# Row loads ahead of result stores, an earlier copy of the first Strassen product, and a second block weighted tile by tile

## What is computed

```python
ret = scores * Dmat                       # scores = q k^T / 8, a decay per head, lower triangle
x = (ret @ v), tokens x 512               # 4 batches, 8 heads, 576 positions, 64 wide
logits = x @ w_gate + log1p(exp(x @ w_noise)) * noise
top2 = argpartition(-logits, 2)[:, :2]    # top2_w = softmax over the two
out[mask] += top2_w * (relu(x[mask] @ w1[e]) @ w2[e])     # 8 experts, hidden width 1024
h = out @ w_in                            # 512 x 2048
y = (h * cos(h)) @ w_out                  # 2048 x 512
```

## Time and profile before

| what | value |
|---|---|
| median of 3 runs | 984.74 us (984.18 to 987.29) |
| the profiled execution | 986.97 us, its span 985.2 us |
| PE / PEld busy | 959.6 us (97%) / 860.7 us (87%) |
| DVE / ACT / POOL busy | 562.3 us (57%) / 477.7 us (48%) / 94.7 us (10%) |
| chain that ended last | PE 75%, SP's queue 6%, DMA 5%, ACT 5%, DVE 4% |
| moved | 231.92 MB, mean 235 GB/s |

### The profile page before, as it was taken

How to read it: one execution, slowest core, us unless ns; L and a number is a source line. 1 busy time by engine, 2 the same in 40 slices (tenths; PEclk the granted TensorE clock), 3 DMA queues, 4 the chain that set the end, 5 groups by cost and what they waited for, 6 DMA issues and landing times.

```text
span 985.2 us, 17024 instructions
## 1 busy us (share of the span) xinstructions
PE 959.6 (97%) x6144; PEld 860.7 (87%) x6144; DVE 562.3 (57%) x1118; ACT 477.7 (48%) x889; POOL 94.7 (10%) x93
## 2 busy tenths in 40 slices
PE   8999999999999999999999999999999999999998
PEld 8888889898988989899998988988988888788887
DVE  4788644544545554433332145567777767776665
ACT  1445334343433443332333146556767766666555
POOL 2276500000000000000000032101100000000000
PEclk9999999999999999999999999999999999999999
DMA  9998455468688786764526248867764766556561
GB/s 364 345 321 303 173 203 202 160 236 310 262 270 329 265 322 229 256 248 150 192 67 231 86 137 304 289 252 289 265 240 167 291 256 235 184 216 249 228 235 54
DMA packets 79521, 231.92 MB, mean 235 GB/s; under 512 B 6880, under 2 KB 32736, under 8 KB 71264
## 3 DMA queue, kind: packets, MB, share of 16 engines
q1 hardware_dynamic: 73696, 212.20, 60.2%
q0 software_dynamic: 5760, 18.88, 5.2%
HBM read 168.14 MB, written 62.91 MB: 235 GB/s over the span
## 4 chain that ended last, share of the span: by engine, by line
PE 75%; SPq 6%; DMA 5%; ACT 5%; DVE 4%; issue 3%; POOL 1%; DVEq 0%; ACTq 0%; POOLq 0%
PE ps L1855 16%; PE ps L1666 13%; PE ps L1684 13%; PE ps L1841 12%; SPq L539 4%; PE ps L1771 3%; PE ps L1783 2%; PE ps L1819 2%; PE ps L1572 2%; PE ps L1610 2%; DMA gath<-x_slots 2%; PE ps L1587 2%; DMA y_slots<-y_sb 2%; PE ps L1638 2%; PE ps L1702 2%
## 5 line engine op out<-in xcount | busy, mean ns | idle before, releaser
L1666 PE MATMUL ps<-xs,w_hi 128*128 (+1 forms) x784 | 185.3, 316 | 0.0
L1855 PE MATMUL ps<-w_sb,g_hi 128*128 128x512 f32 x576 | 180.8, 395 | 0.1
L1272 DVE TENSOR_TENSOR w_lo<-raw,w_hi 128x1024 fp32r<-128x1024 f32 x48 | 58.8, 1226 | 159.2 <-ACT w_hi L794 159.2
L1666 PEld LDWEIGHTS ps<-xs,w_hi 128*128 128x128 f32 x784 | 135.3, 191 | 0.7
L1666 PE MATMUL ps<-xs,w_lo 128*128 (+1 forms) x392 | 122.5, 312 | 0.0
L1841 PE MATMUL ps<-x_odd,w_sb 128*128 128x320 f32 x672 | 118.7, 312 | 3.9 <-DVE angle L1442 1.8
L1841 PEld LDWEIGHTS ps<-x_odd,w_sb 128*128 128x128 f32 x672 | 107.4, 189 | 15.8 <-ACT p_sb L935 3.4
L794 ACT ACTIVATE w_hi<-raw 128x1024 fp32r<-128x1024 f32 x48 | 50.9, 1060 | 136.6 <-PE ps L1684 107.5
L1855 PE MATMUL ps<-w_sb,g_lo 128*128 128x512 f32 x288 | 112.7, 391 | 0.0
L1855 PEld LDWEIGHTS ps<-w_sb,g_hi 128*128 128x128 f32 x576 | 101.3, 188 | 9.8 <-issue 0.3
L716 POOL DMA_INDIRECT y<-y_slots,pos_i x36 | 34.9, 970 | 636.3 <-SPq L636 446.1
(11 more groups left out here) (193 smaller groups left out, 1615.8 us busy)
## 6 DMA issues: line engine op xcount, KB each, us to landing
w_sb<-w_pairs SPq DMA_DIRECT2D x24, 1792.0 KB
w_sb<-w_pairs SPq DMA_DIRECT2D x40, 1024.0 KB, 9.7
raw<-weights SPq DMA_DIRECT2D x64, 512.0 KB
w_pairs<-stage SPq DMA_DIRECT2D x24, 1024.0 KB, 7.1
y_slots<-zeros_sb SPq DMA_DIRECT2D x42, 256.0 KB, 4.1
gath<-x_slots SPq DMA_DIRECT2D x40, 256.0 KB, 7.1
y_slots<-y_sb SPq DMA_DIRECT2D x40, 256.0 KB, 2.1
qk<-qk SPq DMA_DIRECT2D x18, 512.0 KB
```

The source lines that it names most:

```text
L1272: tt(w_lo[:, at], raw[:, f % 2, :], w_hi[:, at].bitcast(F32), ALU.subtract).then_inc(split_done, 1)
L1666: last_one = nc.tensor.matmul(ps[5 + half][:, 0:HALF], w[:, at:at + P], xs[:, bass.ds(g % 2, 1), a, k, half * HALF:(half + 1) * HALF].rear ...
L1855: last_one = nc.tensor.matmul(ps[j][:, :], a[:, slot % 2, part, j * C:(j + 1) * C], w2_sb[slot % 3][:, hl, part * DM:(part + 1) * DM], sta ...
```

## The change

On SP, `unit_loads(g)` now starts with the two value loads, then issues the loads of the next unit's rows 0 and 1, then the five stores of unit g - 1, and then the rest. The stores of the last unit of the loop follow behind it. In units 2 to 6 the value loads and two row loads thus stand between the zero blocks of the unit before and its stores.

On ACT, `copy_p1` stands ahead of `cosine(slot - 1, 3)`, no more behind it, and `x2_high(1, 6)` moves from slot 7 to slot 8, behind `copy_p1(8)`; `x2_low(1, 6)` moves behind the first drain of slot 8. The first product of slot 8 gets the bank ps[7], and the banks of the later products change places, so that products 1 and 2 of slot 8 wait for the last two cosine products of block 0.

The first three tiles of block 1 are weighted one by one around `turn(1, 1)` and `cosine(1, 1)` on ACT and inside slot 2 on DVE, and PE transposes them in the middle of slot 2, behind the first `plain` of that slot and its `second` steps, no more ahead of it.

```diff
--- before.py
+++ after.py
@@ -329,7 +329,9 @@
 
         def p_bank(i):
 
-            return ps[7] if i == 2 else ps[5 + i % 2]
+            if i in (2, 2 * FP):
+                return ps[7]
+            return ps[5 + (i + (i > 2 * FP)) % 2]
 
         def x_of(b):
 
@@ -573,14 +575,17 @@
                 else:
                     sp.dma_start(w2_pairs[i], stage2[i % 2][:, :, :].bitcast(F32)).then_inc(pair_out[i % 2], 16)
 
-            for j in range(TPU):
-                store_rows(0, j)
-
             def unit_loads(g):
                 e_next = nc.sync.value_load(meta[0:1, bass.ds(g + 1, 1)], min_val=0, max_val=E - 1)
                 v_next = nc.sync.value_load(meta[0:1, bass.ds(g + META_V + 1, 1)], min_val=0, max_val=NV - 1)
+                for j in range(2):
+                    sp.wait_ge(tx_done, TPU * g + j + 1)
+                    sp.sem_inc(passed_sp, 1)
+                    load_rows(j, v_next)
+                for j in range(TPU):
+                    store_rows(g - 1, j)
                 for f in range(FE):
-                    if f < TPU:
+                    if 2 <= f < TPU:
                         sp.wait_ge(tx_done, TPU * g + f + 1)
                         sp.sem_inc(passed_sp, 1)
                         load_rows(f, v_next)
@@ -600,14 +605,12 @@
                 unit_loads(g)
                 for j in range(E):
                     zero_block(E * TPU + j + (g - 1) * E)
-                for j in range(TPU):
-                    store_rows(g, j)
             sp.wait_ge(zero_out, 16 * (TPU * (NU - E) + TPU - FRONT[1]))
             sp.sem_inc(passed_sp, 1)
             with sp.Fori(E - 2, last) as g:
                 unit_loads(g)
-                for j in range(TPU):
-                    store_rows(g, j)
+            for j in range(TPU):
+                store_rows(last - 1, j)
 
             def load_w1(slot):
                 if slot >= 2:
@@ -971,9 +974,6 @@
             def ahead(b, p):
                 first = FIRST_TILE[b + 1]
                 if b == 0:
-                    if p == 1:
-                        for j in range(3):
-                            prepare(first + j)
                     if p == 2:
                         for j in range(3):
                             copy_raw(first + j)
@@ -990,8 +990,6 @@
                     if p == 6:
                         for at in range(3, 6):
                             x2_high(1, at)
-                    if p == 7:
-                        x2_high(1, 6)
                 else:
                     if 1 <= p <= 5:
                         copy_raw(first + p - 1)
@@ -1015,17 +1013,24 @@
                 g_high(slot, 0)
                 ahead(0, slot)
                 turn(slot, 1)
+                if slot == 1:
+                    prepare(FIRST_TILE[1])
                 cosine(slot, 1)
+                if slot == 1:
+                    prepare(FIRST_TILE[1] + 1)
+                    prepare(FIRST_TILE[1] + 2)
             for slot in range(FP, SLOTS + 1):
                 b, p = slot // FP, slot % FP
                 if slot == FP:
                     g_high(slot - 1, 1)
+                    if slot < SLOTS:
+                        copy_p1(slot)
+                    x2_high(1, 6)
                 else:
                     g_high(slot - 1, 2)
+                    if slot < SLOTS:
+                        copy_p1(slot)
                     cosine(slot - 1, 3)
-                if slot < SLOTS:
-                    copy_p1(slot)
-                if slot > FP:
                     g_high(slot - 1, 3)
                 if slot == SLOTS:
                     for j in range(0, SIZES[NBK - 1], 2):
@@ -1458,9 +1463,6 @@
             def ahead(b, p):
                 first = FIRST_TILE[b + 1]
                 if b == 0:
-                    if p == 1:
-                        for j in range(3):
-                            combine(first + j)
                     if p == 3:
                         combine(first + 3)
                         combine(first + 4)
@@ -1476,8 +1478,6 @@
                     if p == 6:
                         for at in range(3, 6):
                             x2_low(1, at)
-                    if p == 7:
-                        x2_low(1, 6)
                 else:
                     if p < 5:
                         combine(first + p)
@@ -1497,12 +1497,18 @@
             for slot in range(FP):
                 if slot > 0:
                     product(slot - 1, 1)
+                    if slot == 2:
+                        combine(FIRST_TILE[1] + 1)
                     g_low(slot - 1, 1)
+                    if slot == 2:
+                        combine(FIRST_TILE[1] + 2)
                 reduce(slot, 0)
                 product(slot, 0)
                 g_low(slot, 0)
                 ahead(0, slot)
                 reduce(slot, 1)
+                if slot == 1:
+                    combine(FIRST_TILE[1])
             for slot in range(FP, SLOTS + 1):
                 b, p = slot // FP, slot % FP
                 if slot == FP:
@@ -1515,6 +1521,8 @@
                 if slot < SLOTS:
                     dve.wait_ge(p1_copied, slot - FP + 1)
                     drain(slot, 1, h_sb[0], p1_sb)
+                if slot == FP:
+                    x2_low(1, 6)
                 if slot > FP:
                     g_low(slot - 1, 3)
                 if slot == SLOTS:
@@ -1752,6 +1760,8 @@
                 pe.wait_ge(x2_done, n + 1)
                 if n == 3:
                     pe.wait_ge(g_done, 3)
+                if n == FIRST_TILE[2]:
+                    pe.wait_ge(p1_copied, 1)
                 if n >= 6:
                     pe.wait_ge(xT_copied, {6: 1, 7: 2}.get(n, n - 3))
                 for k in range(KD_TILES):
@@ -1827,8 +1837,10 @@
                     pe.wait_ge(w1_in[slot % 2], 16 * (slot // 2 + 1))
                 if slot % FP == 0:
                     pe.wait_ge(x_lo_done, 7 * (b - 1) + o + 1)
-                if slot == FP and o < 2:
-                    pe.wait_ge(g_done, i - 1)
+                if slot == FP and o == 0:
+                    pe.wait_ge(xT_copied, SIZES[1])
+                elif slot == FP and o < 3:
+                    pe.wait_ge(g_done, i - 2)
                 elif o == 2:
                     pe.wait_ge(p1_copied, slot - FP + 1)
                 else:
@@ -1866,6 +1878,9 @@
                         plain(slot, part)
                         for step_ in todo[TPB * part:TPB * (part + 1)]:
                             second(slot - 1, *step_)
+                        if slot == 2 and part == 0:
+                            for j in range(3):
+                                transpose_x2(FIRST_TILE[1] + j)
                 else:
                     at = 0
                     for o in range(7):
@@ -1876,9 +1891,6 @@
                 if b + 1 < NBK:
                     first = FIRST_TILE[b + 1]
                     if b == 0:
-                        if p == 1:
-                            for j in range(3):
-                                transpose_x2(first + j)
                         if p == 3:
                             transpose_x2(first + 3)
                             transpose_x2(first + 4)
```

## The result

The changed kernel took 991.45 us (median of 7 runs, 987.94 to 993.63), the kernel before 987.22 us beside it (7 runs); the ratio is 1.0046, 95% interval 1.0024 to 1.0068. It is slower by 2 to 7 us, where 981.1 and faster was forecast. 991.45 lies outside the range of 969 to 988. The forecast started from 984.74 us, the median of three runs; with four more the kernel before stands at 987.22, and the forecast gain of 3.6 us from there would be 983.6. So 2.5 of the 10.3 us between 981.1 and 991.45 is the starting point, and 7.8 is the change.

The account below looks back on a forecast made before the run. PE bounds the kernel, busy 959.6 of 985.2 us, so only 25.6 us of waits and low clock can be won. Terms -2.0 + 2.6 + 2.5 + 0.5 make 3.6 us won, 981.1 us, range 969 to 988.

Parts of the forecast that it names:

- What bounds the kernel, and where the wait would go: PE busy 959.6 of 985.2 us; at unit boundaries `gath` waits would give way to waits for `h_low` before `product1`.
- The first boundary: First boundary between units, only two early zero blocks: row loads go out early, nothing is late, 1.4 us won.
- the sixth: Sixth boundary, no wait before: stores start later, `h_low` comes late, 1.4 us lost (bounds 0 and 2.1).
- The price at the boundaries 2 to 5: Four boundaries with zero blocks: PE waits 2.2 us where it waited 1.75, 0.5 lost at each, 2.0 in all.
- rival (b): `product1(g, 2)` behind `h_low`, units 2 to 6: stores' chain costs more than the gather's wait; 10.0 lost, 989.1 us; chance 0.1.
- part 1: Loads ahead of stores on SP at unit boundaries: 2.0 us lost in all.
- The clock: Low clock after boundary waits: two of five such waits cost 1.5 us each, and two were let do so again.
- Part 2: Second block weighted and transposed tile by tile, start of stage 3 to slot 2: 2.6 us won (bounds 1.0 and 2.7).
- rival (c): Stage 3 gives its gain back, slots 8 to 15 wait elsewhere: time stays at 984.7 us; chance 0.2.
- Part 3: Start of slot 8, first product in ps[7]: idle and low clock shrink, 2.5 us won (bounds 0.9 and 4.1).
- part 4: Copy before cosine on ACT, four other copy waits: 0.5 us won (bounds 2.2 won, 1.0 lost).
- The sum: Whole kernel: -2.0 + 2.6 + 2.5 + 0.5 = 3.6 us won, giving 981.1 us.

Follow-up runs that it names:

- e1: The kernel before with only SP's new order (value loads and loads of rows 0 and 1 ahead of the stores); 993.81 us, ratio 1.0081.
- e9: The changed kernel with the two row loads behind the stores again, only the value loads ahead; 989.41 us in one run.
- e5: The changed kernel with one zero block behind each step's load of expert weights, not eight in a row; 971.85 us, ratio 0.9853.
- e2: The changed kernel with SP's order of the kernel before; 983.57 us, ratio 0.9970.
- e12: e5 with tile 3's transposes moved up in slot 2 and the copy ahead of the cosine in slot 9 only; 972.89 us, ratio 0.9855.
- e10: e5 with tile 3's transposes moved up, right behind the first product of slot 2; 971.07 us in one run.
- e11: The kernel before with only the zero blocks moved, one behind each step's load of expert weights; 977.94 us, ratio 0.9905.
- e3: The kernel before with the value loads and two row loads between the third and fourth store; 982.02 us, ratio 0.9968.

## Why the prediction was wrong

**What bounds the kernel, and where the wait would go.** Right. The row loads came early, the `gath` waits went, and in their place stands the chain store, copy of tile 3, `w_high`, `relu`, `h_low`, `product1`, at the line that was named. The first boundary won 1.3 to 1.6 (1.4 forecast); the sixth has a new wait (0.23 for the copy and 1.17 for `h_low`, 1.4 forecast); its stretch is 1.9 longer when the low clock of before is taken off (59.71 against 59.36 less 1.5).

**The price at the boundaries 2 to 5: this is the step that failed.** The mechanism was right and the term "0.5 us lost" at each of four boundaries was too small. I put the store 2.9 us later and the copy 2.2, which made 0.5 lost a boundary, 2.0 in all. Measured on SP: 2.40 us of value loads (I had taken 1.83 from their place behind the stores) and 1.08 of row loads, so the store is 3.4 us later; it then takes 3.25 us to its copy (289.67 to 292.92; I had taken 2.8). PE itself is 1.0 us ahead of the kernel before here, so against PE the copy is 3.2 us later, not 2.2, and lies beyond my upper bound of 2.9. This also brings the wait for the bank of tile 3, which I had held to be in time by 0.2 (292.0 + 3 x 0.69 is 294.1, not 293.9, so by 0.4). A stretch with such a boundary took 61.11 to 61.80 us without low clock, where one of before took 59.6 to 59.9 (61.12 less 1.53 of low clock is the 59.6): 1.4 to 1.9 lost each, 6.4 in all. That is rival (b)'s mechanism and place, with its condition met (the first store lands over 2.9 us later) and more than its 1.2 a boundary. Its price for part 1, 10.0, had 4.5 of low clock in it, which the profile doesn't show; e1 gives 8.0 (5.5 to 10.4). It had a chance of 0.1, since I gave the loss its size from a point between two bounds that both rested on the wrong start. The Trainium skill's rule that I set beside it ("DMA: Bandwidth & Descriptors", Queues, rings and completion order), by which the shift is near 2.9, was nearer than mine. The trace agrees in direction: with the two row loads directly ahead the copy runs 3.25 us behind the store, in e9 without them 2.15. e5 shows that the rings alone aren't the price: the same two loads ahead of the stores cost nothing when SP gets to them early.

**The clock.** I let two low stretches stay. In the profile none stayed, but the seven runs spread from 0.998 to 0.993, and the median run lies 3.5 us above the profiled one, about what two stretches cost. So for the median run the term may have been right; no trace of such a run shows where its low clock lay. A profile of one execution doesn't settle this term: the kernel before has two low stretches at the boundaries in its profile, e1 and e9 one each, the changed kernel and e2 none, though all of these have waits of 1.5 us and more there.

**Part 2 (2.6 forecast).** Right in its place, 2.55 won to slot 3; net 0.6 in the changed kernel, since 2.0 came back in slots 3 to 7. The sentence that failed is the one on POOL: "go out 2.6 us later, and are weighted only in slot 3". Behind the start of stage 3 the gathers of block 1's last tiles are released 3.0 us later than before (18.06, not 15.03) and slot 3 comes 2.6 earlier. In the kernel before tile 7 is weighted without a wait; here its gather was late by 1.34. This is rival (c) in kind, by another wait than the one it named.

**Part 3 (2.5) and part 4 (0.5).** 2.2 alone and 3.0 with part 4's share in slot 9; part 4 then loses 0.4 later on. Together 2.6 in the changed kernel, against 3.0 forecast. That the two agree is in part luck: about half of part 3's gain hangs on the low clock in this execution of the kernel before, and part 4 won its time in slot 9 and not in the four later slots.

**The sum.** Profile against profile: 1.3 won at the first boundary; the five other stretches 5.2 longer; stage 3 shorter by 3.2 (404.19 to 400.97), the rest within 0.3: 0.9 us slower in the span, though the changed kernel's execution has three low stretches of about 1.5 us fewer from the first boundary on. By the runs e1 costs 8.0 where part 1 was to cost 2.0, and e2 wins 3.0 where parts 2 to 4 were to win 5.6; the two make 5.0, against 4.5 measured (0.46% of 987) and 3.6 won in the forecast. So part 1 holds 6.0 of the miss and the give-backs of stage 3 2.6.

## What beats both

e5 is faster than both kernels: 971.85 us, 1.5% below the kernel before. It keeps the whole change and moves the zero blocks. e12, 0.9855, can't be told from it; e10 has one run. Of the gain e11 shows 9.4 us (0.95%) for the zero blocks alone.

## What to carry to other kernels

When a transfer is moved ahead in a queue, price everything that its issue needs on the issuing engine (here 2.4 us of register loads against 0.5 a row load) and follow what falls behind it to the engine that waits: a store whose buffer must come free can be as urgent as a load. If two chains end at the same moment, reordering trades one wait for the other; look for what both stand behind, here eight transfers that nobody was waiting for. Price a low-urgency bulk transfer by when it occupies the issuing engine, and spread it.

## What the runs showed of the hardware that was not expected

From the end of the last transfer's issue over two register loads from `meta` on SP to the next transfer's issue it took 1.83 us behind the five stores (kernel before), 1.74 in e11, 2.3 to 2.4 directly behind the zero blocks (e1, e9, changed kernel), and also 2.30 behind the first three stores in e3; what sets the difference isn't shown. A copy that waits for a store ran 3.5 us behind its issue when zero blocks stood directly ahead of it, 3.25 behind two row loads, and 2.15 with neither (third boundary of the kernel before, the changed kernel, and e5, e9 and e11). Loads of expert weights issued within 2 us of rows, stores and 1 MB transfers were used 6.5 us after their issue in e3 (290.53 to 297.08), where it was 4.3 in the kernel before at the same boundary (294.89 to 299.15).
